# Three pairs of PSUM banks for the scores and one output bank in an attention that feeds two MLPs

## The reference

```python
batch, n_heads, seq, head_dim = 2, 12, 448, 64
scores = q @ k.T / sqrt(64)                      # per batch and head
scores = cap * tanh(scores / cap)                # cap = 30
attn = exp(scores - rowmax); attn /= attn.sum(-1) + 1e-9
x = (attn @ v)                                   # heads side by side: 896 x 768
x = relu(x @ w_in1) ** 2 @ w_out1                # 768 -> 2048 -> 768
out = silu(x @ w_in2) @ w_out2                   # 768 -> 2048 -> 768, 896 x 768 f32
```

## Time and profile before

| | |
|---|---|
| median of 3 runs | 581.03 us (580.96 to 581.09) |
| the profiled execution | 581.64 us, its span 579.8 us |
| granted TensorE clock over the span | 0.999 |
| busy: PE, DVE, ACT, POOL | 568.9, 222.6, 167.3, 82.5 us |
| attention: steady slots | 25.62 to 101.78 us |
| end of the last output product of the attention | 109.85 us |

### The profile page before, as it was taken

The page is one execution under the profiler, slowest core; times in us unless marked ns, Lnnn a source line. Parts: engine busy times, 40 slices in busy tenths (PEclk is TensorE's granted clock), DMA queues, the critical chain, the costliest instruction groups (busy, mean ns, idle before and its releaser), DMA issues.

```text
span 579.8 us, 7548 instructions
## 1 busy us (share of the span) xinstructions
PE 568.9 (98%) x2780; PEld 469.8 (81%) x2780; DVE 222.6 (38%) x355; ACT 167.3 (29%) x207; POOL 82.5 (14%) x54
## 2 busy tenths in 40 slices
PE   7899999999999999999999999999999999999996
PEld 6233333799999999999999999999999999999995
DVE  2189897754444445212111213333333402120210
ACT  2988899032222222202120113222222211110100
POOL 0798989400000000000000000000000000000000
PEclk9999999999999999999999999999999999999999
DMA  7997410011111122121212011111112212121553
GB/s 173 226 223 197 138 53 27 28 56 54 54 54 54 54 72 72 37 72 36 72 36 63 27 55 54 55 54 54 54 54 72 71 39 66 43 61 49 94 86 48
DMA packets 81970, 41.93 MB, mean 72 GB/s; under 512 B 26656, under 2 KB 78880, under 8 KB 81952
## 3 DMA queue, kind: packets, MB, share of 16 engines
q1 hardware_dynamic: 80800, 41.12, 27.8%
q10 hardware_dynamic: 1120, 0.57, 0.5%
q0 software_dynamic: 32, 0.00, 0.0%
HBM read 38.93 MB, written 2.75 MB: 72 GB/s over the span
## 4 chain that ended last, share of the span: by engine, by line
PE 97%; POOL 1%; ACT 1%; issue 0%; DVE 0%; POOLq 0%; ACTq 0%
PE ring L364 14%; PE ring L366 14%; PE ring L365 14%; PE o_t L364 13%; PE o_t L366 13%; PE o_t L365 13%; PE ring L308 5%; PE o_t L320 5%; PE o_t L327 2%; PE ring L305 2%; PE o_t L318 1%; PE ring L354 1%; ACT prob L460 0%; POOL asum L276 0%; POOL asum L269 0%; POOL asum L272 0%
## 5 line engine op out<-in xcount | busy, mean ns | idle before, releaser
L686 DVE TENSOR_TENSOR w_lo<-w_raw,w_hi 128x768 fp32r<-128x768 f32 (+1 forms) x56 | 63.4, 1132 | 297.5 <-ACT w_hi L488 297.5
L488 ACT ACTIVATE w_hi<-w_raw 128x768 fp32r<-128x768 f32 (+1 forms) x56 | 52.4, 937 | 359.9 <-PE ring L366 184.0
L364 PE MATMUL ring<-x_hi,w_hi 128*128 128x448 f32 x384 | 140.7, 366 | 0.0
L366 PE MATMUL ring<-x_hi,w_lo 128*128 128x448 f32 x384 | 140.5, 366 | 0.0
L365 PE MATMUL ring<-x_lo,w_hi 128*128 128x448 f32 x384 | 140.5, 366 | 0.0
L365 PE MATMUL o_t<-g_lo,w_hi 128*128 128x448 f32 x384 | 140.2, 365 | 0.0
L364 PE MATMUL o_t<-g_hi,w_hi 128*128 128x448 f32 x384 | 140.2, 365 | 0.0
L366 PE MATMUL o_t<-g_hi,w_lo 128*128 128x448 f32 x384 | 140.2, 365 | 0.0
L364 PEld LDWEIGHTS ring<-x_hi,w_hi 128*128 128x128 f32 x384 | 72.1, 188 | 7.6 <-issue 1.4
L366 PEld LDWEIGHTS ring<-x_hi,w_lo 128*128 128x128 f32 x384 | 72.1, 188 | 6.2
L365 PEld LDWEIGHTS ring<-x_lo,w_hi 128*128 128x128 f32 x384 | 72.1, 188 | 6.2
(11 more groups left out here) (42 smaller groups left out, 269.2 us busy)
## 6 DMA issues: line engine op xcount, KB each, us to landing
w_raw<-in_moe_w_in_dram SPq DMA_DIRECT2D x32, 384.0 KB, 3.3
w_raw<-in_moe_w_out_dram SPq DMA_DIRECT2D x24, 512.0 KB, 3.9
qk_raw<-in_k_dram SPq DMA_DIRECT2D x48, 112.0 KB, 3.0
qk_raw<-in_q_dram SPq DMA_DIRECT2D x44, 112.0 KB, 2.9
out_dram<-rows SPq DMA_DIRECT2D x46, 56.0 KB, 2.2
v_t<-in_v_dram SPq DMA_DIRECT2D x4, 288.0 KB, 6.3
v_t<-in_v_dram SPq DMA_DIRECT2D x4, 192.0 KB, 4.1
qk_raw<-in_q_dram ACTq DMA_DIRECT2D x4, 112.0 KB, 4.5
```

What stands on the lines that cost most here:

```text
L364: pe.matmul(dst, w_hi[par][:, kk, :], mov_hi, start=start, stop=False)
L366: return pe.matmul(dst, w_lo[par][:, kk, :], mov_hi, start=False, stop=stop)
L488: act.activation(w_hi[n.par][:, 0:blocks, :], w_raw[n.par][:, 0:blocks, :], ACT.Copy).then_inc(s_w_hi, 1)
L686: dve.tensor_tensor(w_lo[n.par][:, 0:blocks, :], w_raw[n.par][:, 0:blocks, :], w_hi[n.par][:, 0:blocks, :].bitcast(F32), ALU.subtract).the ...
```

## The change

- PSUM is one tensor of 8 banks. The scores use three pairs of banks in turn (`RING` = 3, counted over all units), the output has one bank (`o_ps`, bank 6) and the sums have one (`d_ps`, bank 7). A unit waits for the tanh of the unit three before it.
- TensorE's order becomes: all four score units of pair j, then all four value products and the sums of pair j - 1.
- `v_x` gets a place for each head with zeros in the other head's 64 rows, so the product of the last unit uses all 128 rows, like the other values.
- `finish(j - 1)` in place of `finish(j - 2)` stands in VectorE's slot, and the values of pair j wait for the product (L610) of pair j - 1 where they waited for that of pair j - 2.
- In `finish`, the addition of epsilon and the subtraction for `x_lo` are written as `scalar_tensor_tensor`, with the same results.
- The additions of pair 0 move from GpSimd to VectorE (`add_first`).
- At the start, SyncE issues k of pair 0 and of pair 1 and then v without a wait between them, and ScalarE's queue issues q of both pairs.
- ScalarE's loop over the pairs is written out.

The core of the diff:

```diff
-            v_x = sb(att, "v_x", [P, PAIRS, D])
+            v_x = sb(att, "v_x", [P, PAIRS, 2, D])
...
-        ring2 = [ctx.enter_context(nc.psum_tensor(f"ring{i}", [P, 2, 512], F32)) for i in range(2)]
-        o_t = [ctx.enter_context(nc.psum_tensor(f"o_t{i}", [P, 2, 512], F32)) for i in range(2)]
-
-        ring = [ring2[i // 2][:, i % 2, :] for i in range(4)]
-        y_ps = [o_t[i // 2][:, i % 2, :] for i in range(4)]
+        banks = ctx.enter_context(nc.psum_tensor("banks", [P, 8, 512], F32))
+        RING = 3
+        o_ps, d_ps = banks[:, 2 * RING, 0:S], banks[:, 2 * RING + 1, 0:S]
+        ring = [banks[:, i, :] for i in range(4)]
+        y_ps = [banks[:, 4 + i, :] for i in range(4)]
...
+        def score_bank(j, u, h=0):
+
+            return 2 * ((C * j.n + u) % RING) + h
...
-            load_part(At(0, 0), 0, k_v, s_first_in[0:2])
-            sp.wait_ge(s_first_in[0], 2 * DMA)
-            load_qk(At(0, 1))
+            load_part(At(0, 0), 0, k_v, s_first_in[0])
+            load_part(At(0, 1), 0, k_v, s_qk_in[1])
             load_v(0)
...
-                    add_units(At(0, j))
+                    if j > 0:
+                        add_units(At(0, j))
             with pool.Else():
-                for j in range(2):
-                    add_units(At(0, j))
+                add_units(At(0, 1))
                 two_steps(pool, 2, PAIRS - 2, add_units)
...
-                if u < CW:
-                    wait(pe, s_ring, C * j.no + (CW - 1 if u == 2 else u - 1))
+                wait(pe, s_ring, C * j.n + u - RING + 1)
                 for h in range(2):
                     rp = slice(D * h, D * h + D)
                     if u == CW:
-                        last = pe.matmul(ring[2 * (u % 2)][rp, 0:S], qk_f[j.par][rp, MAIN:S], qk_f[j.par][rp, S:2 * S],
-                                         start=True, stop=True)
+                        last = pe.matmul(banks[rp, score_bank(j, u), 0:S], qk_f[j.par][rp, MAIN:S],
+                                         qk_f[j.par][rp, S:2 * S], start=True, stop=True)
                     else:
-                        last = pe.matmul(ring[2 * (u % 2) + h][:, 0:S], qk_f[j.par][rp, u * P:u * P + P], qk_f[j.par][rp, S:2 * S],
-                                         start=True, stop=True)
+                        last = pe.matmul(banks[:, score_bank(j, u, h), 0:S], qk_f[j.par][rp, u * P:u * P + P],
...
             def values(j, c):
 
                 for h in range(2):
-                    out_h = o_t[j.par][D * h:D * h + D, 0, 0:S]
                     if c == CW:
-                        rp = slice(D * h, D * h + D)
-                        pe.matmul(out_h, v_x[rp, j.n, :], prob[j.par][rp, 2 * CW, :], start=False, stop=True)
+                        stat, mov = v_x[:, j.n, h, :], prob[j.par][:, 2 * CW, :]
                     else:
-                        pe.matmul(out_h, v_t[:, 2 * j.n + h, c * D:c * D + D], prob[j.par][:, 2 * c + h, :],
-                                  start=(c == 0), stop=False)
+                        stat, mov = v_t[:, 2 * j.n + h, c * D:c * D + D], prob[j.par][:, 2 * c + h, :]
+                    pe.matmul(o_ps[D * h:D * h + D, :], stat, mov, start=(c == 0), stop=(c == CW))
...
             def sums(j):
 
-                pe.wait_ge(s_sum, 4 * j.no + 4)
+                if j.n == 0:
+                    pe.wait_ge(s_sum_first, 4)
+                else:
+                    pe.wait_ge(s_sum, 4 * j.n)
                 for h in range(2):
-                    last = pe.matmul(o_t[j.par][D * h:D * h + D, 1, 0:S], ones[:, :], asum[j.par][:, h, :],
+                    last = pe.matmul(d_ps[D * h:D * h + D, :], ones[:, :], asum[j.par][:, h, :],
                                      start=True, stop=True)
                 last.then_inc(s_att, 1)
 
-            def output_main(j):
+            def output(j):
                 if j.n in V_PARTS:
                     pe.wait_ge(s_v_in[V_PARTS.index(j.n)], 8 * DMA)
-                wait(pe, s_norm, j.no - 1)
-                pe.wait_ge(s_exp, 2 * j.no + 1)
+                wait(pe, s_norm, j.n)
+                pe.wait_ge(s_exp, 2 * j.n + 1)
                 values(j, 0)
                 values(j, 1)
-                pe.wait_ge(s_exp, 2 * j.no + 2)
+                pe.wait_ge(s_exp, 2 * j.n + 2)
                 values(j, 2)
-
-            def slot(j):
-                scores(j, 0)
-                scores(j, 1)
-                output_main(j + -1)
-                scores(j, 2)
-                scores(j, CW)
-                values(j + -1, CW)
-                sums(j + -1)
+                values(j, CW)
+                sums(j)
...
-            pe.wait_ge(s_fill, 1)
-            for u in range(C):
-                scores(At(0, 0), u)
-            for j in range(1, PAIRS):
-                slot(At(0, j))
+            pe.wait_ge(s_fill, 3)
+            for j in range(PAIRS):
+                for u in range(C):
+                    scores(At(0, j), u)
+                if j > 0:
+                    output(At(0, j - 1))
...
-            output_main(At(0, PAIRS - 1))
-            values(At(0, PAIRS - 1), CW)
-            sums(At(0, PAIRS - 1))
+            output(At(0, PAIRS - 1))
...
+            for j in range(2):
+                for h in range(2):
+                    for a in range(2):
+                        at = QB * D + BL * (1 - a)
+                        rp = slice(D * h + BL * a, D * h + BL * a + BL)
+                        act.dma_start(qk_raw[j][rp, at:at + QB * D],
+                                      q_v[j, h]).then_inc(s_first_in[1] if j == 0 else s_qk_in[1], DMA)
...
-            weights(At(0, 1))
-            two_steps(act, 2, PAIRS - 4, weights)
-            weights(At(0, PAIRS - 2))
+            for j in range(1, PAIRS - 1):
+                weights(At(0, j))
...
+                dve.memset(v_x[D * (1 - h):D * (2 - h), :, h, :], 0.0).then_inc(s_fill, 1)
...
-                dve.transpose(den_r[:, :], o_t[j.par][:, 1, 0:S]).then_inc(s_den, 1)
+                dve.transpose(den_r[:, :], d_ps).then_inc(s_den, 1)
                 dve.wait_ge(s_den, 4 * j.no + 1)
-                dve.tensor_scalar(den[:, :], den_r[:, :].rearrange("p (b i) -> p b i", i=BL)[:, :, 0],
-                                  eps_t[:, 0:1], None, ALU.add).then_inc(s_den, 1)
+                part = den_r[:, :].rearrange("p (b i) -> p b i", i=BL)[:, :, 0]
+                dve.scalar_tensor_tensor(den[:, :], part, eps_t[:, 0:1], part,
+                                         op0=ALU.add, op1=ALU.max).then_inc(s_den, 1)
                 dve.wait_ge(s_den, 4 * j.no + 2)
                 dve.reciprocal(den[:, :], den[:, :]).then_inc(s_den, 1)
                 dve.wait_ge(s_den, 4 * j.no + 3)
                 dve.transpose(rinv[:, :].rearrange("p (b i) -> p b i", i=BL),
                               den[:, :].unsqueeze(2).to_broadcast([P, QB, BL])).then_inc(s_den, 1)
                 dve.wait_ge(s_den, 4 * j.no + 4)
-                dve.tensor_tensor(att_o[:, :], o_t[j.par][:, 0, 0:S], rinv[:, :], ALU.mult).then_inc(s_norm, 1)
+                dve.tensor_tensor(att_o[:, :], o_ps, rinv[:, :], ALU.mult).then_inc(s_norm, 1)
                 dve.wait_ge(s_norm, j.no + 1)
                 dve.tensor_copy(x_hi[:, bass.ds(j.no, 1), :], att_o[:, :].unsqueeze(1)).then_inc(s_x_hi, 1)
                 dve.wait_ge(s_x_hi, j.no + 1)
-                dve.tensor_tensor(x_lo[:, bass.ds(j.no, 1), :], att_o[:, :].unsqueeze(1),
-                                  x_hi[:, bass.ds(j.no, 1), :].bitcast(F32), ALU.subtract).then_inc(s_x, 1)
+                dve.scalar_tensor_tensor(x_lo[:, bass.ds(j.no, 1), :], att_o[:, :].unsqueeze(1), 1.0,
+                                         x_hi[:, bass.ds(j.no, 1), :].bitcast(F32),
+                                         op0=ALU.mult, op1=ALU.subtract).then_inc(s_x, 1)
...
-                finish(j + -2)
+                finish(j + -1)
+
+            def add_first():
+
+                t, a = prob[0], asum[0]
+                dve.wait_ge(s_exp, 1)
+                dve.tensor_tensor(a[:, :, :], t[:, 0:2, :], t[:, 2:4, :], ALU.add).then_inc(s_sum_first, 1)
+                dve.wait_ge(s_exp, 2)
+                dve.wait_ge(s_sum_first, 1)
+                dve.tensor_tensor(a[:, :, :], a[:, :, :], t[:, 4:6, :], ALU.add).then_inc(s_sum_first, 1)
+                for h in range(2):
+                    rp = slice(D * h, D * h + D)
+                    dve.wait_ge(s_sum_first, 2)
+                    dve.tensor_tensor(a[rp, h, :], a[rp, h, :], t[rp, 2 * CW, :], ALU.add).then_inc(s_sum_first, 1)
...
             shift(At(0, 0))
-            prepare(At(0, 2))
-            shift(At(0, 1))
+            add_first()
+            slot(At(0, 1))
             two_steps(dve, 2, PAIRS - 4, slot)
             slot(At(0, PAIRS - 2))
             shift(At(0, PAIRS - 1))
             weight_low(At(0, 0), KC)
-            finish(At(0, PAIRS - 3))
+            finish(At(0, PAIRS - 2))
```

(42 more changed lines are left out.)

## The result

The changed kernel takes 587.82 us at the median of four runs (587.42 to 587.90) against 581.00 before: ratio 1.0116, 95% interval 1.0098 to 1.0133. It is slower by 6.8 us, where 575.7 was predicted.

What follows compares the result with a forecast made beforehand. TensorE's own instructions were taken to bound ten of eleven attention slots and the MLPs. Terms -3.7 - 0.3 - 1.9 + 0.4 = -5.5 gave 575.5, rounded up to 575.7 us; own range 574.8 to 576.8, 8-in-10 range 574.6 to 579.8.

Steps and rivals of the forecast that it cites:

- the price of the new forms: VectorE's scalar_tensor_tensor operations in finish: 0.24 and 0.63 us, free of GpSimd; release 2.6 after the sums, 3.35 available.
- the transposes, due at 7.25: VectorE, behind the output bank's release: transposes of the pair after next ready at 5.5 us, at worst 8.6.
- The rest of the slot: TensorE, ten attention slots: fewer changes of array shape, 7.25 us a slot instead of 7.62, -3.7 us in all.
- ScalarE's wait: Before the last pair: two weight copies delay tanh, so score 3 waits 0.45 us; +0.4 us, once.
- the same waits, and slower: Rival: finish waits behind GpSimd, the whole 1.0 us pause stands in each slot, +10, 585.7 us; chance 0.10.
- a rule that covers both instructions: Trainium skill, cited against the forecast: VectorE instructions with two SBUF inputs contend with GpSimd instructions reading SBUF.
- the half price: Rival: waits behind GpSimd stay, but the pause settles near 0.5 us per finish, +5.0, 580.7 us; chance 0.12.
- The start: Before the steady slots: they begin at 23.75 instead of 25.62, -1.9 us; rival that it gives nothing, 577.6, chance 0.06.
- The pause: TensorE at the start, before score 3 of pair 1: a new pause of 2.8 us, waiting for ScalarE's tanh.
- their cover: Loads at the start: 1.7 us of delay covered between pair 0's transposes and the end of TensorE's warm-up; cost 0.
- The last pair: Attention's end, behind the first hidden tile: 3.90 us instead of 4.20, -0.3 us.
- The MLPs: Both MLPs, 465.05 us: bound by TensorE, untouched by the diff except for bank numbers; no term given.

Runs made afterwards that it cites:

- experiment 8: Changed kernel with the epsilon addition's second tensor read from PSUM instead of SBUF (computes the larger of two sums): 577.85 us, ratio 0.9955.
- experiment 1: Changed kernel without the addition of epsilon, the reciprocal reading the transposed sums directly: 576.41 us, ratio 0.9905.
- experiment 3: Changed kernel without the epsilon addition and with x_lo written as zeros by a memset, VectorE's loop written out: 577.53 us, ratio 0.9927.
- experiment 12: Changed kernel without epsilon, with six idle TensorE products in the starting pause and the first MLP's second-product loop written out: 575.83 us, ratio 0.9905.
- Experiment 6: Changed kernel with six idle TensorE products in front of score 3 of pair 1, in the starting pause: 583.80 us, ratio 1.0049.
- run 5: The changed kernel again, unedited, on another chip than its old-forms variant: 584.86 us (583.70 to 587.62), ratio 1.0070.
- run 7: The kernel before without the epsilon addition: 580.85 us, ratio 1.0002.
- run 11: The kernel before with TensorE's loop of the first MLP's second product written out: 581.14 us, ratio 1.0003.
- run 2: Changed kernel with x_lo written as zeros by a memset instead of the subtraction, VectorE's loop written out: 582.90 us, ratio 1.0016.
- run 4: Changed kernel with the epsilon addition and x_lo back in their old forms (tensor_scalar, tensor_tensor): 583.27 us, ratio 1.0037.

## Why the prediction was wrong

**The step that failed** is the price of the new forms: "I take the lower, because the steps of a single stream beside it never wait". The addition was put at 0.24 us and took 1.09 at the median and up to 1.89. It has two streams in SBUF, and experiment 8 shows what that costs by taking one away. The reason given was weak on its own rows, too: the cast is a single stream and took up to 2.24, and so was the old addition, at up to 2.03. The same price failed a second time behind the release: the transposes, due at 7.25, were put at 5.5 and "at worst 8.6", which leaves the small addition at its least; they were ready at 8.8 in every second slot. The rest of the slot was right: 7.26 for 7.25 forecast, as soon as that addition is gone or reads PSUM (experiments 1, 3, 8, 12).

The forecast is 11.3 us below the profiled execution (576.1 against 587.42). The ten slots make 8.1 of it (-3.3 forecast, with ScalarE's wait, +4.8 measured), the MLPs 2.3 and the start 1.0.

**The rival.** It came as "the same waits, and slower": release at 4.2 after the sums where 4.37 was worked out, slots of 8.1 on the mean in the changed kernel where 7.25 + 1.0 was. It gave 585.7 and had a chance of 0.10, too little with a finish of 4.32 us read in the earlier trace rows and a rule that covers both instructions. What it left open, whether GpSimd moves up and halves the price, has two answers: 7.77 with the clock kept, which is the half price, and 8.1 with the fall, which comes near the full one.

**The start** was mis-sized: -1.9 forecast, -0.9 measured. The pause was right (2.8 forecast, 2.58), and its clock was given no price of its own. Experiment 6 puts the fall at 1.4 us in the start, and its profile beside run 5's has the slots in the better beat where the clock is kept. The first transposes began at 7.64, 0.2 later than before and inside their cover, as forecast.

**The last pair** came as forecast (-0.3), and so did ScalarE's wait before the last scores (0.29 for 0.45). `w_lo` wasn't forecast to be late, and was, by 0.47, behind a late `finish`.

**The MLPs** were held to be untouched. The program is, but the profiled run has 2.3 us more there: a term put at nothing. The slower cadence is no accident of one run. Ten of the eleven profiles of the new order have it (all but run 1's: 485 or 486 products in 235 to 335, against 495), and none of the three profiles of the old order. Of the 95 executions of the old order (runs 7 and 11 among them), 7 took 582.8 to 583.2 and the rest at most 581.7, so it seems to come there too, but seldom. So the slower cadence goes with the new order, and what in it brings it on no run here shows. Taking the cadence (2.3) and the fall (1.4 and about 2) off the 587.8 leaves 582, an estimate: even without these two, the waits behind GpSimd cancel the gain.

**What stays open:** what sets the cadence, and whether the length of the pause is all that decides on the clock. It fell in the three profiles whose pause was 2.58 to 2.66 us (the changed kernel twice, and run 1), and not in the four with 1.68 to 2.12 (runs 2, 3, 4 and 8), where TensorE had waited 0.5 to 0.9 us for the transposes of pair 1 just before.

## What to carry to other kernels

Before a buffer is halved, write out the chain from its last writer to its release with each step's longest time, not its least, and look at which engine the neighbour will be adding on at that very moment. A 14-column operation can hold two engines. On a short path, price each VectorE operation by its longest time beside GpSimd, not by counting its inputs: here a second input moved to PSUM ended the wait, but operations with one tensor input from SBUF had waited as well. If the operation can go, it goes. A new pause of TensorE can have a price beyond its length: that of 2.6 us had, those of up to 2.1 us had not.

## What the runs showed of the hardware

- An operation on 14 columns took 0.236 us with one input in SBUF and one in PSUM, and up to 1.89 with both in SBUF, beside the same GpSimd additions (`eps_t`, one value per partition, was in SBUF in both).
- One tensor input was no protection: `tensor_scalar` on 14 columns took 0.23 to 2.12 us (run 4), and the cast on 448 columns 0.39 to 2.24 (kernel before). The reciprocal (0.24) and the transposes had no such spread.
- The granted clock fell to 0.50 (1.2 GHz) behind a pause of TensorE of 2.6 us, in three profiles of three, after it had been busy from 2.19 us on. Near the end of the kernel before it was still at 1.00 three microseconds after the last matmul, which had made me give the new pause no price.
- A stream of products without a gap had two cadences over 576 products, 4 ns apart, at a granted clock of 1.00: the slower in ten of eleven profiles of the new order and in none of three of the old. The loop's form doesn't explain it.
- With two engines in each other's way, slots didn't settle on one length: they alternated (8.97 and 7.26, or 8.0 and 7.5). Runs 5 and 6, which differ in the start alone, have one pair each.
